# Thin and long MLP tasks in alternation over the border between two batches

## The chip, the cores and the metric

The kernel runs on one core of one Trainium2 chip. Its time is the device time of that core in microseconds (us). The engines are named as the profile names them: PE is TensorE's matrix multiply, PEld its weight load, DVE is VectorE, ACT is ScalarE, POOL is GpSimd, and SP is SyncE, which issues most transfers.

## The reference, cut to what matters

Three models in a row, all in float32:

```python
# attention, 4 batches x 8 heads, 576 rows, head size 64
scores = scale * q @ k.T
scores = where(scores >= max(scores) - tau, scores, -1e9)
x = softmax(scores) @ v                      # joined to x[b, 576, 512]
# mixer MLP, one batch after the other
u  = x + (U, V applied over the 576 rows of x)   # rank 32
z  = u + relu(u @ w_ch1) @ w_ch2             # 512 -> 2048 -> 512
# routed experts
logits = z @ w_gate; local_gate = sigmoid(z @ w_local)
e = argmax(logits), or the row before's expert if local_gate >= 0.5
out = softmax(logits)[e] * (relu(z @ w1[e]) @ w2[e])
```

## The kernel before, in words

**Two streams in one loop.** The attention works on pairs of heads (16 pairs, four to a batch), and each pair takes nine steps. Step n therefore belongs to pair p = n // 9, with j = n % 9. Steps 0 to 35 (batch 0) run alone. From step 36 on the MLP of the batch before is woven in: `FILL[n]` lists the MLP tasks of step n. The attention ends with step 143; the steps after it hold only MLP tasks, three to a step. Then comes the routing of all rows to experts, and the experts.

**The tasks.** `mlp_tasks` writes the order of the 82 tasks of a batch. The 576 rows are cut in two stretches, k = 0 with 256 and k = 1 with 320, and the 2048 hidden values in four quarters r. A task computes one bank of PSUM:

- `token_mix`: one task, the first rank-32 product. `mixed` (k, c): the second product plus x, giving u in four blocks c of 128 channels.
- `hidden` (k, r, q): 12 matmuls over u. `channel` (k, r, c): 12 matmuls over the quarter's hidden values, added to z. These are the long tasks; a batch has 32 of each kind, sixteen per k.
- `gate` (k), `logits` (k): the router's products and their transposes. `rows` (i): the five row blocks of z, transposed for storing.

`gate`, `logits`, `rows` and `mixed` are the thin tasks. In the order before, all of a batch's long tasks are done, then `gate` and `logits` of both k, three `rows`, the next batch's `token_mix`, the last two `rows`, and the eight `mixed`, and then the next `hidden`.

**Two banks.** Task t writes bank t % 2 of `mlp_banks`. TensorE waits before task t until ACT and DVE have emptied bank t % 2 of task t - 2 (L663, L664). `hidden` is emptied by ACT (L839) and then DVE (L976), `channel` by DVE (L984), `mixed` by two ACT copies (L836, L837) and DVE (L973), `gate` by ACT (L844), `logits` by DVE (L989), `rows` by ACT (L851). Further waits: `gate` waits for the last `channel` of its k (L699), the first `hidden` of a k for all `mixed` of that k (L682).

**The order on each engine in step n**, written out by hand (L740 to L765, L887 to L913, L1017 to L1038):

- PE: scores of step n + 1 (after ACT's copy `et_copied` of step n - 1), now and then the value product, `turn_out` or `turn_part`, the first MLP task, `turn(n)`, the other MLP tasks.
- ACT: exponential and limit of n + 1, denominators (j = 3, 8), the first task's copy, `copy_turned(n)`, `copy_out` and `copy_part` at some j, the other tasks' copies.
- DVE: minimum and mask of n + 1, `inverse` and `write_x` at j = 1 and 5, then all tasks of the step.

The weight pieces of the MLP pass through a ring of six, which POOL splits (L468, L473) when the last user of a slot is done; the steps for this (`SPLIT_AT`) and for the first expert's weights (`FIRST_LOAD`, `FIRST_UPPER`) follow from the task order.

Of the kernel before, what the change touches and what calls it, by code (L numbers as in the profile page):

```python
# [4 lines left out]
F32 = mybir.dt.float32  # L5
# [21 lines left out]
SCALE = DH ** -0.5  # L27
ROWS = [P] * (NT - 1) + [REST]
# [21 lines left out]
SPLIT_ROWS = 3  # L50


def mlp_tasks():

    tasks = []
    for b in range(B):
        rows = [(b, "rows", 0 if i < BLOCKS[0][1] else 1, i, 0) for i in range(NT)]
        tasks.append((b, "token_mix", 0, 0, 0))
        if b:
            tasks += waiting  # L60
        tasks += [(b, "mixed", k, 0, c) for k in range(2) for c in range(KC)]
        for r in range(NQ):
            for k in range(2):
                tasks += [(b, "hidden", k, r, q) for q in range(QUARTER)]
                tasks += [(b, "channel", k, r, c) for c in range(KC)]
        tasks += [(b, "gate", k, 0, 0) for k in range(2)]
        tasks += [(b, "logits", k, 0, 0) for k in range(2)]
        tasks += rows[:SPLIT_ROWS]
        waiting = rows[SPLIT_ROWS:]
    return tasks + waiting  # L70


TASKS = mlp_tasks()
# [5 lines left out]
def emptied(by, t):  # L79

    return sum(by[:t + 1])


def tasks_by_step():
# [3 lines left out]
    for n in range(ALONE, NBLK):  # L88
        b, at = divmod(n, ALONE)
        if b == 1:  # L90
            want = 0 if at == 0 else 1 if at == 1 else 3 if at in (6, 15, 17, 26) else 2
        else:
            want = 4 if at == 0 else 3 if at in (3, 5, 6, 8, 15, 17, 24, 26) else 2
        plan.append(list(range(done, done + want)))
        done += want
    assert done == INDEX[B - 2, "channel", 1, NQ - 1, KC - 1] + 1
# [41 lines left out]
SPARE = 80  # L138


def attention_and_mlp(nc, ctx, keep, A, first_weights):
# [18 lines left out]
    o_cols = sb("o_cols", [P, PAD])  # L160
    u4 = sb("u4", [P, NT, 4, RANK])
    v4 = sb("v4", [P, S], F32R)
    stat = sb("stat", [P, 4, 2])
# [13 lines left out]
    w_gate = sb("w_gate", [P, KC, P // KC])  # L177
# [4 lines left out]
    g4 = hid_hi[:, 0:2, :].rearrange("p a b -> p (a b)")[:, 0:D]  # L182
# [98 lines left out]
    CLEARS = 17  # L281
# [142 lines left out]
    def gpsimd(pool):  # L424
        done = 0
        for buf in (raw_q[0:REST, :, NT - 1, 1], raw_q[REST:P, :, NT - 1, 0], raw_k[REST:P, :, NT - 1], ident[:], first_k[DH:P, 0:2].bitcast(F32), first_k[0:DH, 2:4].bitcast(F32),
                    raw_v[REST:P, 0, NT - 1], raw_v[REST:P, 1, NT - 1], ex[:, :, S:PAD], u4[REST:P, NT - 1], x[REST:P, NT - 1], gates[:], w_gate[:], z[:, KC * S:], o_cols[:, S:PAD], least[:], den[:]):
# [121 lines left out]
    def tensor(pe):  # L549
# [101 lines left out]
        def turn_out(p, k):  # L651
            pe.wait_ge(o_copied, 2 * p + k + 1)
            for n, c in enumerate(range(*BLOCKS[k])):
                last = nc.tensor.transpose(aux[:, 512 * k + n * P:512 * k + (n + 1) * P], o_cols[:, c * P:(c + 1) * P], ident[:])
# [1007 lines left out]
```

## Time and profile before

| | |
|---|---|
| median of 3 runs | 1121.52 us (1120.58 to 1122.43) |
| the profiled execution's own time | 1121.17 us |
| its span, first to last instruction | 1119.4 us |
| PE busy | 1052.2 us, 94% of the span |
| DVE, ACT, POOL busy | 512.8, 469.2, 367.9 us |
| mean granted TensorE clock | 0.982 of full speed |
| chain that ended last | 85% PE, 4% ACT, 3% DVE, 3% DMA |

A task's time on PE is best read from start to start: the ends of matmuls are modelled and overlap the next start. Border 1 is the stretch in which batch 0's MLP ends and batch 1's begins, border 2 and border 3 the next two. Borders 1 and 2 lie in the part with attention (steps 72 to 78 and 108 to 114); border 3 (steps 144 to 150) and the end of the MLP (steps 171 to 174) lie after it.

### The profile page before, as it was taken

To read this page: it belongs to the slowest core of one execution; us is meant where nothing else is said; L and a number is where in the kernel's file an instruction comes from. 1 tells how busy PE (TensorE), PEld (TensorE's weight loads), DVE (VectorE), ACT (ScalarE), POOL (GpSimd) and SP (SyncE) were. 2 spreads that over 40 slices of the span, in tenths; PEclk is the share of its full clock that TensorE was granted. 3 is DMA by queue.
4 is the path that set the end of the run, shared out by engine and by line. 5 is a ranking of instruction groups with operands and counts; after the bars stand their busy time and mean duration, and the time that the engine had idled before them with its cause. 6 is when DMAs were issued, how large, how long until landed. Compare 5 with 4: busy or idle time off the path is not lost.

```text
span 1119.4 us, 19936 instructions
## 1 busy us (share of the span) xinstructions
PE 1052.2 (94%) x7054; PEld 917.3 (82%) x7055; DVE 512.8 (46%) x1000; ACT 469.2 (42%) x894; POOL 367.9 (33%) x340
## 2 busy tenths in 40 slices
PE   6999899999889999988999998999869999999995
PEld 5766889999679999967999996999757887887784
DVE  4665544545444454545445452222463543335731
ACT  5776534444554443455444343122213442334620
POOL 4455122643403264340326422378110121111111
PEclk9999999999999999999999999999959999999998
DMA  7887051614434361543325113331254533245510
GB/s 165 194 184 186 20 138 46 169 60 118 145 74 95 93 166 49 128 139 80 80 86 144 49 37 120 122 132 39 71 179 142 187 122 124 72 154 185 183 42 31
DMA packets 110649, 127.26 MB, mean 114 GB/s; under 512 B 67213, under 2 KB 67213, under 8 KB 110544
## 3 DMA queue, kind: packets, MB, share of 16 engines
q1 hardware_dynamic: 104480, 114.54, 36.0%
q0 software_dynamic: 3520, 10.75, 3.0%
q8 instruction: 63, 1.03, 0.4%
q10 hardware_dynamic: 2544, 0.59, 0.2%
q14 instruction: 42, 0.34, 0.1%
HBM read 87.90 MB, written 10.22 MB: 88 GB/s over the span
## 4 chain that ended last, share of the span: by engine, by line
PE 85%; ACT 4%; DVE 3%; DMA 3%; issue 3%; SPq 1%; POOL 1%; POOLq 0%; ACTq 0%; DVEq 0%
PE mlp_banks L696 18%; PE mlp_banks L688 18%; PE p_down L1353 11%; PE p_up L1353 8%; PE aux L646 7%; PE score_banks L622 6%; PE score_banks L629 6%; DMA xg<-mlp_rows,gather_at 2%; PE p_turn L1373 1%; PE aux L589 1%; PE p_x L1346 1%; DMA mlp_rows<-z_rows 1%; ACT et_first L814 1%; DVE stat L928 1%; PE mlp_banks L671 1%
## 5 line engine op out<-in xcount | busy, mean ns | idle before, releaser
L788 ACT ACTIVATE ex<-score_banks,stat 128x576 f32<-128x576 f32 x132 | 97.8, 741 | 178.0 <-DVE stat L928 178.0
L468 POOL CAST w_hi<-stage 128x1024 fp32r<-128x1024 f32 x64 | 66.6, 1041 | 288.2 <-PE mlp_banks L688 240.8
L688 PE MATMUL mlp_banks<-u_hi,w_hi 128*128 128x320 f32 (+1 forms) x512 | 157.0, 307 | 3.7 <-ACT u_hi L837 3.3
L696 PE MATMUL mlp_banks<-hid_hi,w_hi 128*128 128x320 f32 (+1 forms) x512 | 158.5, 310 | 0.9 <-DVE hid_lo L976 0.9
L937 DVE SCALAR_TENSOR_TENSOR ex<-score_banks,stat,ex 128x576 f32<-128x576 f32 x132 | 107.7, 816 | 106.6 <-ACT stat L792 105.7
L473 POOL TENSOR_TENSOR w_lo<-stage,w_hi 128x1024 fp32r<-128x1024 f32 (+1 forms) x70 | 154.0, 2202 | 4.8
L688 PE MATMUL mlp_banks<-u_hi,w_lo 128*128 128x320 f32 (+1 forms) x512 | 151.3, 296 | 0.0
L696 PE MATMUL mlp_banks<-hid_lo,w_hi 128*128 128x320 f32 (+1 forms) x512 | 151.3, 296 | 0.0
L696 PE MATMUL mlp_banks<-hid_hi,w_lo 128*128 128x320 f32 (+1 forms) x512 | 151.3, 296 | 0.0
L688 PE MATMUL mlp_banks<-u_lo,w_hi 128*128 128x320 f32 (+1 forms) x512 | 151.3, 295 | 0.0
L1353 PE MATMUL p_down<-weights,hid_upper 128*128 x336 | 111.9, 404 | 5.7 <-issue 5.7
L1353 PE MATMUL p_up<-weights,x_upper 128*128 x336 | 111.7, 404 | 3.5 <-issue 1.8
L976 DVE SCALAR_TENSOR_TENSOR hid_lo<-mlp_banks,hid_hi 128x256 fp32r<-128x256 f32 (+1 forms) x128 | 58.4, 456 | 113.4 <-ACT hid_hi L839 112.8
L928 DVE TENSOR_REDUCE stat<-score_banks 128x1 f32<-128x576 f32 x132 | 99.4, 753 | 22.9 <-PE score_banks L622 14.2
L839 ACT ACTIVATE hid_hi<-mlp_banks 128x256 fp32r<-128x256 f32 (+1 forms) x128 | 52.3, 409 | 135.4 <-PE mlp_banks L688 134.9
L984 DVE TENSOR_TENSOR z<-mlp_banks,z 128x256 f32<-128x256 f32 (+1 forms) x128 | 58.4, 457 | 110.5 <-PE mlp_banks L696 110.5
L622 PE MATMUL score_banks<-k_tiles,q_tiles 128*128 128x288 f32 x552 | 98.0, 303 | 7.9 <-ACT et_first L814 5.4
L696 PEld LDWEIGHTS mlp_banks<-hid_hi,w_hi 128*128 128x128 f32 x512 | 96.8, 189 | 6.1 <-issue 3.3
L688 PEld LDWEIGHTS mlp_banks<-u_hi,w_hi 128*128 128x128 f32 x512 | 96.8, 189 | 5.2 <-ACT u_hi L837 3.5
L1294 POOL DMA_INDIRECT out<-x,scatter_at x21 | 21.5, 1022 | 234.7 <-DVE x L1575 234.7
L696 PEld LDWEIGHTS mlp_banks<-hid_lo,w_hi 128*128 128x128 f32 x512 | 97.0, 190 | 0.0
L688 PEld LDWEIGHTS mlp_banks<-u_lo,w_hi 128*128 128x128 f32 x512 | 97.0, 190 | 0.0
(231 smaller groups left out, 1950.4 us busy)
## 6 DMA issues: line engine op xcount, KB each, us to landing
stage<-in_moe_w_ch SPq DMA_DIRECT2D x64, 512.0 KB, 3.7
w_raw<-in_moe_w SPq DMA_DIRECT2D x64, 512.0 KB, 5.2
q_tiles<-q_parts SPq DMA_DIRECT2D x30, 320.0 KB, 4.3
q_tiles<-q_parts SPq DMA_DIRECT2D x60, 160.0 KB, 4.2
k_tiles<-k_parts SPq DMA_DIRECT2D x60, 144.0 KB, 3.5
raw_q<-in_q SPq DMA_DIRECT2D x32, 128.0 KB, 3.2
raw_v<-in_v SPq DMA_DIRECT2D x32, 128.0 KB, 2.8
raw_k<-in_k SPq DMA_DIRECT2D x28, 128.0 KB, 2.7
```

Of the source, the lines that this page charges most:

```text
L468: nc.gpsimd.tensor_copy(w_hi[:, n % RING], stage[:, n % 2]).then_inc(w_upper, 1)
L473: last = nc.gpsimd.tensor_tensor(w_lo[:, n % RING, cols], stage[:, n % 2, cols], w_hi[:, n % RING, cols].bitcast(F32), ALU.subtract)
L622: last = nc.tensor.matmul(score_of(n)[:, a], q_tiles[:, s, 2 * m + t, i * P:(i + 1) * P], k_tiles[:, s, m, a * HALF:(a + 1) * HALF], start ...
L629: last = nc.tensor.transpose(turned_of(n)[:, c], ex[:, n % 3, c * P:(c + 1) * P], ident[:])
L646: last = nc.tensor.matmul(aux[h * DH:(h + 1) * DH, 512 * k:512 * k + w], raw_v[:, p % 2, c, h], et[k][:, h, c], start=(c == 0), stop=(c == ...
L688: last = nc.tensor.matmul(bank[:, 0:w], ch1(a, g, d, c), of[:, d, cols], start=(d == 0 and n == 0), stop=(d == KC - 1 and n == 2))
L696: last = nc.tensor.matmul(bank[:, 0:w], ch2(a, g, q, c), of[:, q, 0:w], start=(q == 0 and n == 0), stop=(q == QUARTER - 1 and n == 2))
L788: nc.scalar.activation(ex_of(n), score_of(n), ACT.Exp, bias=stat[:, n % 4, 0:1], scale=-1.0).then_inc(exp_done, 1)
L928: nc.vector.tensor_reduce(stat[:, n % 4, 0:1], score_of(n), AX.XY, ALU.min).then_inc(row_min, 1)
L937: nc.vector.scalar_tensor_tensor(out=ex_of(n), in0=score_of(n), scalar=stat[:, n % 4, 1:2], in1=ex_of(n), op0=ALU.is_le, op1=ALU.mult, acc ...
L976: nc.vector.scalar_tensor_tensor(out=hid_lo[:, c, 0:w], in0=bank[:, 0:w], scalar=0.0, in1=hid_hi[:, c, 0:w].bitcast(F32), op0=ALU.max, op1 ...
L1353: last = nc.tensor.matmul(to, a, weights[:, bass.ds(at_w + b + c * step, 512)], start=(c == 0 and k == 0), stop=(c == len(rows) - 1 and k ...
```

## The change

The second half of a batch's last quarter (k = 1, r = 3) is held back. Its four `hidden` take turns with `gate`, `logits` and two `rows` of k = 0; its four `channel` take turns with the next batch's `mixed` of k = 0; and `gate`, `logits` and three `rows` of k = 1 take turns with the next batch's first four `hidden`. In every batch, the batch alone at the start too, the first four `channel` of k = 0 take turns with the `mixed` of k = 1. `g4`, which `token_mix` writes, gets a buffer of its own instead of lying over `hid_hi`. The list of tasks per step changes with it; the MLP has 177 steps in all instead of 175. In batches 1 and 2 of the loop some steps hold three or four tasks (`FIRST_STEPS`). A few pads are not cleared any more (15 instead of 17 clears), the gate's stationary operand has 16 columns per block instead of 32, and the last row block of some transposes 64 rows instead of 128.

For the last batch there is no next one: after its last `hidden` (k = 1, r = 3) with the thin tasks of k = 0 between them come four `channel`, `gate`, `logits` and three `rows`, one after the other.

```diff
-SPLIT_ROWS = 3
+def taking_turns(*lists):
+    return [task for row in itertools.zip_longest(*lists) for task in row if task is not None]
...
-        if b:
-            tasks += waiting
-        tasks += [(b, "mixed", k, 0, c) for k in range(2) for c in range(KC)]
+        tasks += taking_turns(left[:KC], quarter("mixed", 0, 0))
+        tasks += taking_turns(left[KC:], quarter("hidden", 0, 0))
+        tasks += taking_turns(quarter("channel", 0, 0), quarter("mixed", 1, 0))
         for r in range(NQ):
             for k in range(2):
-                tasks += [(b, "hidden", k, r, q) for q in range(QUARTER)]
-                tasks += [(b, "channel", k, r, c) for c in range(KC)]
-        tasks += [(b, "gate", k, 0, 0) for k in range(2)]
-        tasks += [(b, "logits", k, 0, 0) for k in range(2)]
-        tasks += rows[:SPLIT_ROWS]
-        waiting = rows[SPLIT_ROWS:]
-    return tasks + waiting
+                if (r, k) not in ((0, 0), (NQ - 1, 1)):
+                    tasks += quarter("hidden", k, r) + quarter("channel", k, r)
+        tasks += taking_turns([gate[0], logits[0]] + rows[:BLOCKS[0][1]], quarter("hidden", 1, NQ - 1))
+        ends.append(len(tasks))
+        left = quarter("channel", 1, NQ - 1) + [gate[1], logits[1]] + rows[BLOCKS[0][1]:]
+    return tasks + left, ends
...
+FIRST_STEPS = (2, 2, 3, 4, 2, 3, 2, 3, 3, 2, 2, 2)
...
         if b == 1:
-            want = 0 if at == 0 else 1 if at == 1 else 3 if at in (6, 15, 17, 26) else 2
+            want = min(at, 2)
         else:
-            want = 4 if at == 0 else 3 if at in (3, 5, 6, 8, 15, 17, 24, 26) else 2
+            want = FIRST_STEPS[at] if at < len(FIRST_STEPS) else 3 if at in (15, 20, 25, 30) else 2
...
-    o_cols = sb("o_cols", [P, PAD])
+    o_cols = sb("o_cols", [P, S])
+    g4 = sb("g4", [P, D], F32R)
...
-    w_gate = sb("w_gate", [P, KC, P // KC])
+    w_gate = sb("w_gate", [P, KC, GATES])
...
-    CLEARS = 17
+    CLEARS = 15
...
             elif kind == "logits":
+                pe.wait_ge(act_task, emptied(BY_ACT, INDEX[b, "gate", k, 0, 0]))
...
+                if k == 1 and b < B - 1:
+                    act.wait_ge(rows_stored[0], 16 * (3 * b + 1))
+                    act.wait_ge(rows_stored[1], 16 * (2 * b + 1))
                 nc.scalar.copy(gate_part[:, START[k]:START[k] + w], bank[:, 0:w]).then_inc(act_task, 1)
```

The steps of the changed plan that the prediction speaks of, in the kernel's names (b is the batch whose MLP it is; border 1 shown, border 2 is 36 steps later):

```
70 gate k0, hidden k1 r3 c0          77 gate k1, hidden k0 r0 c0 (b+1), logits k1
71 logits k0, hidden c1              78 hidden c1 (b+1), rows 2
72 rows 0, hidden c2                 79 hidden c2, rows 3, hidden c3
73 rows 1, hidden c3                 80 rows 4, channel k0 r0 c0, mixed k1 c0
74 token_mix, channel c0, mixed c0   81 channel c1, mixed k1 c1
75 channel c1, mixed c1, c2, c2      82 channel c2, mixed k1 c2
76 channel c3, mixed c3              83 channel c3, mixed k1 c3; 84 hidden k1 r0 c0
```

## Rows read from the trace of the kernel before

**Rows 1.** PE's waits over the whole span: waited for, us, times, longest

```profile
PE mlp_banks L676 <- ACT z_rows L851: 3.9, 3, 1.7
```

**Rows 2.** Stretch, us; busy PE, PEld, DVE, ACT, POOL; PE clock, DMA share, GB/s

```profile
288.44:323.31 34.87, 27.86 (x190) 20.99 (x190) 14.70 (x34) 20.21 (x49) 7.34 (x6) 0.95 0.56 145
323.31:485.24 161.93, 161.59 (x1238) 150.83 (x1238) 77.96 (x170) 69.20 (x152) 64.23 (x43) 1.00 0.37 98
485.24:518.52 33.28, 26.26 (x190) 20.23 (x190) 14.70 (x34) 20.22 (x49) 7.34 (x6) 1.00 0.57 152
677.76:698.10 20.34, 16.46 (x104) 11.40 (x103) 5.05 (x14) 9.62 (x25) 4.18 (x3) 1.00 0.34 110
```

**Rows 3.** Timeline of PE in border 2, and one value product of border 1

```profile
490.18 0.60 PE L709 MATMUL mlp_banks<-ident,z 128*128 128x128 f32 x4
490.62 0.71 PE L629 MATMUL score_banks<-ident,ex 128*128 128x128 f32 x5
...
494.37 4.46 PE L671 MATMUL mlp_banks<-x,u 128*128 128x512 f32 x10
498.26 1.09 PE L622 MATMUL score_banks<-k_tiles,q_tiles 128*128 128x288 f32 x4
...
503.99 2.38 PE L646 MATMUL aux<-et_first,raw_v 128*64 128x256 f32 x20
506.29 0.39 PE L676 MATMUL mlp_banks<-v,hid_hi 128*128 128x256 f32 x1
...
506.96 0.71 PE L629 MATMUL score_banks<-ident,ex 128*128 128x128 f32 x5
...
307.52 3.64 PE L646 MATMUL aux<-et_first,raw_v 128*64 128x256 f32 x20
```

**Rows 4.** Timeline of PE in a dense step: turn, long task, scores

```profile
571.84 0.71 PE L629 MATMUL score_banks<-ident,ex 128*128 128x128 f32 x5
572.31 0.36 PE L696 MATMUL mlp_banks<-hid_hi,w_hi 128*128 128x256 f32 x1
...
573.82 0.69 PE L622 MATMUL score_banks<-k_tiles,q_tiles 128*128 128x288 f32 x4
574.34 0.28 PE L696 MATMUL mlp_banks<-hid_hi,w_hi 128*128 128x256 f32 x1
```

**Rows 5.** Timeline of a thin step of border 1, all engines

```profile
295.67 0.79 PE L622 MATMUL score_banks<-k_tiles,q_tiles 128*128 128x288 f32 x4 [0.70 <-ACT et_first L814]
...
296.50 0.76 DVE L928 TENSOR_REDUCE stat<-score_banks 128x1 f32<-128x576 f32 x1 [0.35 <-PE score_banks L622]
...
297.29 0.74 ACT L788 ACTIVATE ex<-score_banks,stat 128x576 f32<-128x576 f32 x1 [0.62 <-DVE stat L928]
...
298.25 0.82 DVE L937 SCALAR_TENSOR_TENSOR ex<-score_banks,stat,ex 128x576 f32<-128x576 f32 x1 [0.99 <-ACT stat L792]
298.58 0.71 ACT L814 ACTIVATE et_first<-score_banks 128x640 f32<-128x640 f32 x1
```

**Rows 6.** Timeline without attention: a k = 1 hidden's emptying

```profile
788.68 0.31 PE L688 MATMUL mlp_banks<-u_hi,w_hi 128*128 128x320 f32 x1
...
788.88 0.44 ACT L839 ACTIVATE hid_hi<-mlp_banks 128x320 fp32r<-128x320 f32 x1 [7.25 <-PE mlp_banks L688]
...
789.35 0.49 DVE L976 SCALAR_TENSOR_TENSOR hid_lo<-mlp_banks,hid_hi 128x320 fp32r<-128x320 f32 x1 [1.81 <-ACT hid_hi L839]
```

**Rows 7.** Timeline of the end of the MLP and of the routing

```profile
801.09 1.49 PE L701 MATMUL mlp_banks<-z,w_gate 128*32 128x256 f32 x16
...
804.06 0.32 DVE L1458 TENSOR_REDUCE c<-gates 128x20 f32<-128x160 f32 x1
...
804.13 3.25 ACT L851 COPY x<-mlp_banks 128x512 f32<-128x512 f32 x5 [1.07 <-PE mlp_banks L709]
...
808.89 1.34 DVE L1477 TENSOR_TENSOR_SCAN won<-kept,p_up 32x576 f32<-32x576 f32 x1
```

**Rows 8.** Busy time from 306 to 312 us, columns as in rows 2

```profile
306.00:312.00 6.00, 6.00 (x37) 4.04 (x38) 1.91 (x4) 2.37 (x7) 0.00 (x0) 0.72 0.82 187
```

## The prediction on record

> **What bounds the kernel now.** I read the share of busy time first: PE works 94% of the span, so only PE's own gaps can be won. The list of waits then says where they are: nearly all that are not at the start or in the routing belong to thin tasks around a border, such as `mixed` waiting 3.9 us in three places for a `rows` copy [rows 1]. Third, the windows [rows 2]: between borders 1 and 2 PE is busy 161.59 of 161.93 us, in the three borders 27.86 of 34.87, 26.26 of 33.28 and 16.46 of 20.34. Busy time is flattering, since modelled ends cover part of each gap, so I count work from start to start. A `rows` task takes 0.44 and `token_mix` 3.9 us; the k = 0 value product takes 2.3 and a k = 0 `mixed` 0.67 [rows 3]; in a dense stretch `turn` takes 0.47, a k = 0 long task 1.51 and the scores 0.52 [rows 4]; a k = 1 long task takes 1.76 and a k = 1 `mixed` about 0.76 (320 columns for 256).
>
> Border 2 by these: 6 scores 3.1, 7 turns 3.3, `token_mix` 3.9, value product 2.3, five `rows` 2.2, eight `mixed` 5.7, `gate` and `logits` about 1.9, `turn_out` and `turn_part` about 1.2 (the last two by their counts of matmuls): 23.6 of 33.28 us, so 9.7 are lost. Border 1 has the same work and loses 11.3; 1.3 of the difference is its value product, 3.64 instead of 2.38 us [rows 3], in a stretch whose granted clock is 0.72 on average, partly the 1.2 GHz level [rows 8], behind a gap of 1.7 us on PE [rows 1]. Border 3 has 14.4 of work in 20.34 us and loses 5.9. That is 27 us in sight. The question is how much of it comes back.
>
> **What ends a wait now.** Two chains set the least length of a step. From the scores' start (295.67) it is 0.83 to the minimum, 0.79 to the exponential, 0.96 to the mask's start, 0.82 to its end: 3.40 us, and only then does DVE turn to the step's tasks [rows 5]. ACT comes to a first task's copy 2.45 us after the scores' start and to `copy_turned` after that, which the scores after next need: 3.62 us from the scores' start to that copy's end in this step, with a `rows` copy in front (295.67 to 299.29). Without attention, a k = 1 `hidden` is out of its bank 1.16 us after the next task starts (788.68 to 789.84) [rows 6]; a `channel`, without the ACT copy, 0.69; k = 0 about 1.05 and 0.62. PE's first matmul after a wait costs another 0.1.
>
> **The change, attention borders (1 and 2).** The same tasks and the same matmuls; what alters is the cover. I walk steps 70 to 84 with these durations, each engine in its own order, and note where PE must wait:
> - Steps 70 to 76. `gate` k0 now directly follows the last `channel` of its k: 0.2 beyond the scores that cover it. Steps 71 and 72 are short (3.2 of PE work), so scores wait 0.4 for `copy_turned`. `token_mix` is well covered, its emptying by `channel` c0. Step 75 holds four tasks: `channel` c2 needs `channel` c1 out of its bank, but DVE reaches it only behind the mask, 4.4 after the scores' start, where PE is at 3.6: 0.9.
> - Steps 77 to 80. Each has one or two long tasks with a thin one between, 3.6 to 4.4 us of PE work a step. Scores wait 0.4, 0.3 and 0.7 for `copy_turned`; `hidden` c1 waits 0.3 and c3 0.8 for the `hidden` two tasks before; in step 80 `mixed` waits 0.9 for the `rows` 4 copy, behind exponential, limit and denominators on ACT.
> - Steps 82 to 84. Scores wait 0.3, 0.4 and 0.2, `turn_part` 0.3 for `copy_part`; `channel` c3 waits 0.7 for c2, behind mask and `write_x` on DVE; and `hidden` k1 c0 waits 1.3, because it needs the `mixed` just before it, where before eight long tasks lay between.
>
> That sums to 8.1, with some seven restarts 8.8 us a border, beside 9.7 and 11.3, to which 0.2 is added in both for a wait two steps behind the old borders. Border 2 gains 1.1 and border 1 2.7, if the half clock stays away: **-3.8**. The bounds of a border's loss: 4.6 if the bank waits vanish (then only ScalarE's loop, the `mixed` wait and a few tenths are left), and 10 or more if the DVE queue slips further.
>
> **Border 3, without attention.** Nothing stands between the tasks any more but the tasks. A `hidden` behind a thin task waits for the `hidden` before it: emptying 1.05 to 1.16 plus restart 0.1, minus the thin task's 0.33 to 0.44, so 0.75 to 0.85 each. There are four of these with the next batch's first `hidden` and the following `channel` (0.85 + 3 x 0.75 = 3.1), two more in steps 143 and 145 that `turn` or `turn_out` covers partly (1.0), `hidden` k0 c0 behind `gate` waits 0.8 for `mixed` c3, `hidden` k1 c0 waits 1.7 for `mixed` k1 c3. `channel` beside `mixed` is nearly free (0.69 against 0.67), 0.2, and the change of operand type costs 0.08 on seven long tasks, 0.6. Sum 7.4 beside 5.9: **+1.5**.
>
> **End of the MLP.** Before, `gate` and `logits` of k = 0 fitted into waits that k = 1 has anyway: from 801.09 to the routing's first instruction at 804.06 [rows 7]. This end stays as long. Ahead of it, though, now stand `gate` 0.57, `logits` 0.33 and two `rows` 0.86, which before lay in that wait or behind `logits` under the routing; plus the wait of `gate` for the `channel` just before it 0.8 and three `hidden` waits 1.0 + 0.9 + 0.9, and 0.1: 5.3. Back comes part: ACT has three `rows` copies instead of five (3.25 us from 804.13) ahead of the exponential and copy that the scan at 808.89 waits for, 0.9 [rows 7]. **+4.4**. Bounds: +1.7 if the `hidden` waits were covered, +5.3 if the scan gained nothing.
>
> **Batch 0.** `mixed` k1 moves from steps 40 and 41 to 42 to 45. The old place loses about 2.5 there; the new one has three short steps (3.3 of PE work) with scores waits of 0.25, 0.25 and 0.7, and a `hidden` k1 wait of 0.85, with restarts 2.7: **+0.2**.
>
> **Free parts.** Fewer clears sit before POOL's idle time; 16 instead of 32 stationary columns and 64 instead of 128 change no column that streams; `g4`'s own buffer removes no wait seen. Transfers keep their place relative to their users: a `rows` 2 store has two steps until `rows` 4 needs the buffer, POOL's splits and SP's loads, the experts' first weights too, move together with the last user of their slot. If POOL were late, the next `channel` would show it first.
>
> **Sum.** -3.8 + 1.5 + 4.4 + 0.2 = +2.3 us on the profiled execution's 1121.17 gives 1123.5. The median of the runs is 0.35 above that execution: 1123.8 us.
>
> **A rule weighed.** The two-bank rotation hides an emptying only as long as the task in between: 1.16 us against 0.44 [rows 3, 6]. The Trainium skill, Perfetto Trace Analysis, section Matmuls, says that independent matmul groups should rotate through banks so that the emptying of one overlaps the next group. If that held in full here, all bank waits would go. By rows: 4.6 instead of 8.8 at two borders, 4.1 less at border 3, 2.7 less at the end, so 1108.6 us; I give it 0.05 within the first rival below.
>
> **Rivals.**
> - Faster (0.25): the bank waits at borders 1 and 2 are covered because delayed scores leave DVE time for the step's tasks. Loss 4.6 each, a gain of 12.2 where I count 3.8: 1115.4 us. For it speaks that borders 1 and 2 lose most in waits behind one `rows` copy [rows 1], which long tasks do cover; against it that DVE takes tasks strictly behind the mask. It is faster by over 0.2% from a loss of about 6.5 a border downwards.
> - Slower by more (0.20): the slips of steps 77 to 84 add up, or PE falls to 1.2 GHz in one of them as it did at 306 [rows 8]. The borders lose what they did, and only the +6.1 of the rest stays: 1127.6.
> - Nothing comes of it (0.15): waits only change places, and the end, too, is covered: 1121.5.
> - My forecast (0.40), its own range 1121.8 to 1125.8, half within 0.2% and half above.
>
> **Chances.** 0.2% (2.2 us) is about what a measurement can tell from no change. Faster 0.25; same 0.15 + 0.18 = 0.33; slower 0.22 + 0.20 = 0.42. The range reaches from the faster rival's number to the slower one's, 1115.5 to 1127.5, and leaves about 0.2 out.
>
> **What would show it.** After the change: waits of L688 for `hid_lo` (L976) of 0.7 to 1.0 us around border 3 and at the end; one of over 1 us for `mixed` (L973) before `hidden` k1 in every batch; no wait of `mixed` for a `rows` copy over 1 us, except 0.9 at step 80; border windows from step 70 to 84 with 8 to 9 us more than their work; a clock of 1.00 there; the routing's first instruction at 804.06 + 5.3 + 1.5 + 0.2 - 3.8 = 807.3 us. It is wrong if the borders lose under 6.5 each, or if the end moves the routing by less than 3.

## The result, and the profile after

The changed kernel takes 1127.07 us (median of 20 runs, 1124.96 to 1128.95) beside 1121.84 us for the kernel before (20 runs, 1119.89 to 1127.75): ratio 1.0042, 95% interval 1.0033 to 1.0051. It is slower, by some 4.7 us by the ratio and 5.2 between the medians. The forecast was 1123.8, slower by 2.3, with a range from 1115.5 to 1127.5: the measured time lies at the upper end of it.

The profiled execution has a span of 1124.4 us beside 1119.4, with the same clock over the whole, 0.983 and 0.982. Line numbers have moved: `hidden` is L702 now, `channel` L710, `mixed` L690 and L692, `gate` L715, `logits` L720; the copies are L854 (`hid_hi`), L994 (`hid_lo`), L862 (`gate`) and L869 (`rows`).

PE's waits over the whole span, which answer to [rows 1] (waited for, us, times, longest):

```profile
PE mlp_banks L702 <- DVE hid_lo L994: 3.9, 8, 0.7
PE mlp_banks L702 <- DVE u_lo L991: 3.6, 4, 1.5
...
PE mlp_banks L710 <- ACT u_hi L852: 1.6, 2, 0.8
PE mlp_banks L702 <- ACT x L869: 1.4, 2, 0.7
PE mlp_banks L690 <- ACT z_rows L869: 1.4, 2, 0.7
...
PE mlp_banks L715 <- DVE z L1002: 1.3, 2, 0.7
```

The wait of `mixed` for a `rows` copy has gone from 3.9 to 1.4 us, as the change means it to. The first two rows are what took its place: a `hidden` that wants its bank while DVE still empties the `hidden` two tasks before, and a k = 1 `hidden` that wants the last `mixed`. Where these waits stand is shown by PE's timeline, rows with an idle time only. Border 2 (border 1 is the same 194.2 us earlier):

```profile
493.15 0.39 PE L710 MATMUL mlp_banks<-hid_hi,w_hi 128*128 128x320 f32 x1 [0.79 <-ACT u_hi L852]
...
514.10 0.36 PE L702 MATMUL mlp_banks<-u_hi,w_hi 128*128 128x256 f32 x1 [0.67 <-DVE hid_lo L994]
519.42 0.41 PE L690 MATMUL mlp_banks<-v,g 128*128 128x320 f32 x1 [0.70 <-ACT z_rows L869]
...
537.54 0.38 PE L702 MATMUL mlp_banks<-u_hi,w_hi 128*128 128x320 f32 x1 [0.84 <-DVE u_lo L991]
```

Border 3, without attention (the last row is `hidden` k1 c0 behind `mixed` k1 c3):

```profile
689.83 0.35 PE L702 MATMUL mlp_banks<-u_hi,w_hi 128*128 128x256 f32 x1 [0.69 <-DVE hid_lo L994]
692.52 0.36 PE L702 MATMUL mlp_banks<-u_hi,w_hi 128*128 128x256 f32 x1 [0.58 <-DVE hid_lo L994]
695.21 0.35 PE L702 MATMUL mlp_banks<-u_hi,w_hi 128*128 128x256 f32 x1 [0.59 <-DVE hid_lo L994]
...
709.17 0.38 PE L702 MATMUL mlp_banks<-u_hi,w_hi 128*128 128x320 f32 x1 [1.47 <-DVE u_lo L991]
```

The end of the MLP, PE's timeline, and DVE's for one `hidden`, the routing's first instruction and the scan, which answer to [rows 7]:

```profile
787.16 0.62 PE L715 MATMUL mlp_banks<-z,w_gate 128*16 128x256 f32 x8 [0.61 <-DVE z L1002]
790.88 0.38 PE L702 MATMUL mlp_banks<-u_hi,w_hi 128*128 128x320 f32 x1 [0.92 <-DVE gates L1007]
794.03 0.38 PE L702 MATMUL mlp_banks<-u_hi,w_hi 128*128 128x320 f32 x1 [0.71 <-ACT x L869]
796.53 0.49 DVE L994 SCALAR_TENSOR_TENSOR hid_lo<-mlp_banks,hid_hi 128x320 fp32r<-128x320 f32 x1 [2.65 <-ACT hid_hi L854]
797.17 0.39 PE L702 MATMUL mlp_banks<-u_hi,w_hi 128*128 128x320 f32 x1 [0.70 <-ACT x L869]
806.88 0.73 PE L715 MATMUL mlp_banks<-z,w_gate 128*16 128x320 f32 x8 [0.67 <-DVE z L1002]
808.24 0.52 PE L720 MATMUL mlp_banks<-ident,z_rows 128*128 128x128 f32 x3 [0.63 <-ACT z_rows L862]
...
809.16 0.32 DVE L1476 TENSOR_REDUCE c<-gates 128x20 f32<-128x160 f32 x1
813.10 1.34 DVE L1495 TENSOR_TENSOR_SCAN won<-kept,p_up 32x576 f32<-32x576 f32 x1 [0.48 <-ACT kept L1422]
```

The brackets of the three `hidden` name the event that came last before them, the emptying of the thin task just before. By the program each waits for the `hidden` two tasks before: DVE ends that one's emptying at 797.02 (796.53 + 0.49), and PE starts at 797.17.

The routing begins at 809.16 instead of 804.06 and its scan at 813.10 instead of 808.89. Nearly the whole loss is in place by then.

### The profile page after: what moved, and what is told of

The parts are those of the page before. It is cut to its first block, busy times and chain, and to the rows that moved or that the text cites. A ratio compares the mean times of both kernels' runs of the same rounds, so it can differ in the third digit from the quotient of the medians.

```text
span 1124.4 us, 19937 instructions
## 1 busy us (share of the span) xinstructions
PE 1054.0 (94%) x7054; PEld 917.0 (82%) x7055; DVE 510.7 (45%) x1000; ACT 471.2 (42%) x894; POOL 367.2 (33%) x338
## 4 chain that ended last, share of the span: by engine, by line
PE 78%; SPq 6%; DVE 5%; issue 4%; ACT 4%; DMA 3%; POOL 1%; POOLq 0%; DVEq 0%; ACTq 0%
PE mlp_banks L710 18%; PE mlp_banks L702 17%; PE p_down L1371 11%; PE p_up L1371 8%; PE aux L660 6%; PE score_banks L636 5%; PE score_banks L643 5%; DMA xg<-mlp_rows,gather_at 2%; PE mlp_banks L685 2%; PE p_x L1364 1%; PE p_turn L1391 1%; PE aux L603 1%; DVE stat L946 1%; PE mlp_banks L692 1%; DVE hid_lo L994 1%
## 5 line engine op out<-in xcount | busy, mean ns | idle before, releaser
L702 PE MATMUL mlp_banks<-u_hi,w_hi 128*128 128x320 f32 (+1 forms) x512 | 158.6, 310 | 10.9 <-DVE hid_lo L994 3.9
L710 PE MATMUL mlp_banks<-hid_hi,w_hi 128*128 128x320 f32 (+1 forms) x512 | 158.4, 309 | 3.8 <-ACT u_hi L852 1.6
L702 PE MATMUL mlp_banks<-u_hi,w_lo 128*128 128x320 f32 (+1 forms) x512 | 151.4, 296 | 0.0
L710 PE MATMUL mlp_banks<-hid_hi,w_lo 128*128 128x320 f32 (+1 forms) x512 | 151.3, 296 | 0.0
L702 PE MATMUL mlp_banks<-u_lo,w_hi 128*128 128x320 f32 (+1 forms) x512 | 151.3, 295 | 0.0
L710 PE MATMUL mlp_banks<-hid_lo,w_hi 128*128 128x320 f32 (+1 forms) x512 | 151.2, 295 | 0.0
L994 DVE SCALAR_TENSOR_TENSOR hid_lo<-mlp_banks,hid_hi 128x256 fp32r<-128x256 f32 (+1 forms) x128 | 58.4, 456 | 153.3 <-ACT hid_hi L854 153.0
L854 ACT ACTIVATE hid_hi<-mlp_banks 128x256 fp32r<-128x256 f32 (+1 forms) x128 | 52.4, 409 | 143.3 <-PE mlp_banks L702 143.1
L702 PEld LDWEIGHTS mlp_banks<-u_hi,w_hi 128*128 128x128 f32 x512 | 96.8, 189 | 18.4 <-issue 6.1
L710 PEld LDWEIGHTS mlp_banks<-hid_hi,w_hi 128*128 128x128 f32 x512 | 96.8, 189 | 8.8 <-issue 3.5
L710 PEld LDWEIGHTS mlp_banks<-hid_lo,w_hi 128*128 128x128 f32 x512 | 97.0, 189 | 0.2 <-issue 0.2
L702 PEld LDWEIGHTS mlp_banks<-u_lo,w_hi 128*128 128x128 f32 x512 | 97.0, 189 | 0.0
```

Of the source, the lines that this page charges most:

```text
L702: last = nc.tensor.matmul(bank[:, 0:w], ch1(a, g, d, c), of[:, d, cols], start=(d == 0 and n == 0), stop=(d == KC - 1 and n == 2))
L710: last = nc.tensor.matmul(bank[:, 0:w], ch2(a, g, q, c), of[:, q, 0:w], start=(q == 0 and n == 0), stop=(q == QUARTER - 1 and n == 2))
L994: nc.vector.scalar_tensor_tensor(out=hid_lo[:, c, 0:w], in0=bank[:, 0:w], scalar=0.0, in1=hid_hi[:, c, 0:w].bitcast(F32), op0=ALU.max, op1 ...
```

## How the runs are compared

A row of the timeline says when a piece of work begins, so the stretch between two such rows holds a known set of tasks. I cut each profiled execution at seven rows: the scores that PE computes in step 37 (those of step 38; below and in the expectations "the scores of step 37"); `hidden` k1 r0 c0 of batches 0, 1, 2 and 3 (written h0 to h3); the routing's first instruction; and PE's first gather of rows (`p_x`), behind the routing. Up to h3 the MLP tasks in each stretch are the same for all orders; at the end the new order puts two `rows` ahead of the routing which otherwise lie behind it. The attention's steps in it are the same for all kernels with the changed plan of steps; with the plan of before, one or two steps fall into the stretch beside it. The kernels are described in the two sections on experiments. Stretches in us:

```
                     37-h0   h0-h1   h1-h2   h2-h3  h3-rout.  -p_x   -end
before               43.63  197.78  195.21  170.74   94.27   25.77  289.6
rest_only            43.64  196.24  195.27  170.53   94.28   25.83  289.8
plan_only            44.31  196.60  194.97  169.62   94.34   25.73  289.5
after                44.75  195.74  194.20  171.63   99.99   24.96  290.3
only_end             43.65  196.23  196.80  170.61   99.86   24.97  294.3
end_undone           44.78  195.77  194.24  171.63   94.38   25.83  291.4
border3_end_undone   44.80  195.76  194.22  170.40   94.31   25.83  291.3
mixed_first          44.87  194.31  192.70  170.18   99.96   24.97  292.6
hybrid               44.32  194.30  192.67  171.33   94.30   25.82  292.1
before_banks4        43.67  196.24  195.27  166.94   94.30   25.42  289.7
banks4               44.80  195.75  194.22  167.22   96.92   24.97  289.4
hybrid_banks4        44.31  194.30  192.69  166.01   94.29   25.49  293.2
held3_banks4         44.33  194.31  192.69  165.74   94.42   25.48  289.7
first_banks4         44.89  194.31  192.68  165.70   96.89   24.97  290.9
```

Where two kernels have the same instructions in a stretch, it repeats to a few hundredths (h3 to the routing: 94.27 to 94.42 in the nine kernels with the old end), except for the last column, for two stretches over an old border, 197.78 and 196.80, and for h2 to h3 with the old border 3 (169.6 to 171.3), of which more below.

## Experiments: which part costs what

**The old order with all other edits (`rest_only`).** The order of tasks and the plan of steps are those of before; `g4`'s own buffer, the narrower gate weights and transposes, the fewer clears and the extra wait of `logits` stay (the extra wait of `gate`'s copy for earlier stores goes with the new order). In this and all further kernels `HELD[b]` says whether batch b's last quarter is held back, and `MIX[b]` where batch b's `mixed` of k = 1 go: all ahead (`early`), in turns behind a `channel` (`turns`), or in turns ahead of it (`first`). Against the changed kernel:

```diff
+HELD = (False, False, False, False)
+MIX = ('early', 'early', 'early', 'early')
...
+        else:
+            tasks += waiting + quarter("mixed", 0, 0)
+            if MIX[b] == "early":
+                tasks += quarter("mixed", 1, 0)
+            tasks += quarter("hidden", 0, 0)
+        if MIX[b] == "early":
+            tasks += quarter("channel", 0, 0)
...
+        else:
+            tasks += gate + logits + rows[:3]
+            left, waiting = [], rows[3:]
...
-            want = FIRST_STEPS[at] if at < len(FIRST_STEPS) else 3 if at in (15, 20, 25, 30) else 2
+            want = 4 if at == 0 else 3 if at in (3, 5, 6, 8, 15, 17, 24, 26) else 2
```

> The old order of tasks and the old list of steps, with all other edits of the change (own buffer for g4, 16 stationary columns in the gate, 64 rows in the last transposes, 15 clears). Theory (only the order costs): within 1 us of the kernel before, ratio 0.999 to 1.001, and the routing's first instruction (the reduction over gates) at 804 us as before. Rival (the small edits cost part of it): 2 us or more slower.

Measured: 1122.08 us (12 runs) beside 1122.11, ratio 1.0000 (0.9987 to 1.0013). The free parts are free as far as this interval of 1.5 us each way can tell, and the loss is in the order of tasks or its plan of steps.

**The new end alone (`only_end`).** `rest_only`, but the last batch's `gate`, `logits` and two `rows` of k = 0 take turns with its last quarter of `hidden`.

```diff
-HELD = (False, False, False, False)
+HELD = (False, False, False, True)
```

> As rest_only, but the last batch alone is in the new order at its end: thin tasks of k = 0 between the four hidden of k = 1, then four channel, gate, logits and three rows. Theory (the end is what costs): gate, logits and two rows are put ahead of the routing (1.8 us), one wait of gate and three of hidden for a bank are new (3.6 us), 0.9 us come back in front of the scan: 4.5 to 5 us slower than before, ratio 1.004; the routing's first instruction 5.3 us later than in rest_only. Rival (the end is hidden, the loss sits at the three borders): under 2 us slower.

Measured: 1129.30 us (6 runs), ratio 1.0060 (1.0040 to 1.0081). From h3 to the routing it takes 99.86 us instead of 94.28, and 24.97 instead of 25.83 from there to `p_x`: +5.6 and -0.9. PE's timeline has the waits of the changed kernel, one after the other:

```profile
788.29 0.63 PE L729 MATMUL mlp_banks<-z,w_gate 128*16 128x256 f32 x8 [0.61 <-DVE z L1016]
792.02 0.38 PE L716 MATMUL mlp_banks<-u_hi,w_hi 128*128 128x320 f32 x1 [0.93 <-DVE gates L1021]
795.15 0.38 PE L716 MATMUL mlp_banks<-u_hi,w_hi 128*128 128x320 f32 x1 [0.71 <-ACT x L883]
798.29 0.38 PE L716 MATMUL mlp_banks<-u_hi,w_hi 128*128 128x320 f32 x1 [0.71 <-ACT x L883]
```

The sum, 4.7, is most of the 7.2 us in its median. In its profiled execution 1.5 us more lie in border 2 and 4.5 behind the routing, both in the clock (last sections).

**The end undone (`end_undone`).** The changed kernel with the old end for the last batch.

```diff
+HELD = (True, True, True, False)
+MIX = ('turns', 'turns', 'turns', 'turns')
```

> The changed kernel with the old order at the end of the last batch alone. Theory: 4.5 to 5 us faster than the changed kernel, so level with the kernel before (ratio 0.999 to 1.001). Rival (the loss sits at the borders): still 3 us or more slower than before.

Measured: 1123.12 us (12 runs), ratio 1.0003 (0.9987 to 1.0019). The stretch to the routing is back at 94.38, the next at 25.83. So from both sides the end costs 4.7 us in the stretches; in the times of the runs it is 4.4 by the ratios (1.0042 to 1.0003) and 3.9 between the medians. Without it the change is no longer slower by anything that can be measured. Nor is it faster.

**Border 3 and the end undone (`border3_end_undone`).** Only borders 1 and 2 keep the new order, and the last batch has `mixed` k1 in its old place.

```diff
+HELD = (True, True, False, False)
+MIX = ('turns', 'turns', 'turns', 'early')
```

> The changed kernel with the old order at the end and at border 3, the two stretches without attention; borders 1 and 2 and batch 0 stay new. Theory (alternation pays where attention steps stand between the tasks, and costs where none do): 1.5 to 3 us faster than end_undone, ratio to before 0.997 to 0.9985. Rival (border 3 is even): as end_undone.

Measured: 1121.72 us (12 runs), ratio 0.9993 (0.9980 to 1.0006); h2 to h3 170.40 us instead of 171.63. Border 3 in the new order costs 1.2 us beside this kernel. That is less than the 1.5 to 3 us that I expected, and the ratio is above the expected 0.997 to 0.9985: with `mixed` in turns behind `channel`, the new order at borders 1 and 2 is no gain that the runs can tell.

**The plan of steps alone (`plan_only`).** The old order, put on the steps of the changed plan: each border stands two steps later, and more tasks stand behind the attention's end. By difference, 1.3 us were missing in the account. Against `rest_only`:

```diff
-            want = 0 if at == 0 else 1 if at == 1 else 3 if at in (6, 15, 17, 26) else 2
+            want = min(at, 2)
...
-            want = 4 if at == 0 else 3 if at in (3, 5, 6, 8, 15, 17, 24, 26) else 2
+            want = FIRST_STEPS[at] if at < len(FIRST_STEPS) else 3 if at in (15, 20, 25, 30) else 2
```

> The order of tasks of before with the steps of the changed plan (and all the other edits): every border stands two steps later, and two steps' more tasks stand behind the end of the attention. What the forecast left out costs, by difference, about 1.3 us between batch 2's hidden k1 and batch 3's, beside the attention of two steps that lies in front of that stretch instead of in it. Theory that the plan's shift at the attention's end is this cost: from batch 2's hidden k1 to batch 3's within 0.3 us of border3_end_undone's 170.4 us, which has the same steps and the same order there; and the whole to batch 3's hidden k1, from the scores of step 37, 1 to 2 us longer than the 605.7 us of rest_only, ratio 1.000 to 1.003. Rival that the shift costs nothing and the held quarter is what costs: 605.7 us again, and 169 us or less from batch 2's hidden k1 to batch 3's.

Measured: 1122.87 us (12 runs), ratio 1.0002 (0.9987 to 1.0016). My theory fell, and the rival holds in the main, though its stretch is 169.62 and not the 169 or less that it asked for. From the scores of step 37 to h3 it takes 605.50 us, as `rest_only` does (605.68), and h2 to h3 is not the 170.4 that I expected. The shift costs nothing. The 0.8 us between this and `border3_end_undone`, which has the same tasks and steps there, is mostly one transfer. In `border3_end_undone`, ACT's timeline:

```profile
687.91 0.58 ACT L886 COPY z_rows<-mlp_banks 64x512 f32<-64x512 f32 x1 [2.30 <-DMA mlp_rows<-z_rows]
```

and in `plan_only`:

```profile
688.50 0.58 ACT L886 COPY z_rows<-mlp_banks 64x512 f32<-64x512 f32 x1 [1.58 <-PE mlp_banks L709]
```

The `rows` 4 copy waits for an earlier store to leave its buffer in the one and not in the other; PE's next `mixed` then waits 1.37 instead of 0.65 us. Why that store lands later was not tried. `hybrid` (below) has the same tasks there once more and takes 171.33: its copy waits 2.54 us and its `mixed` 1.61, and behind that wait the clock falls, which takes another 0.75 us (from that `mixed` to h3 20.56 us, beside 19.81 in `plan_only`). PE's row, and the window of the fall (the clock is the third number from the end):

```profile
686.29 0.38 PE L707 MATMUL mlp_banks<-v,g 128*128 128x256 f32 x1 [1.61 <-ACT z_rows L886]
688.00:692.00 4.00, 3.77 (x18) 3.52 (x17) 1.12 (x3) 2.01 (x6) 0.00 (x0) 0.57 0.00 1
```

With `plan_only` the parts can be compared at equal steps, for the order alone: batch 0 +0.44, border 1 -0.86, border 2 -0.77, h2 to h3 +2.01, the end +5.65 and -0.77.

## Experiments: what the waits are made of, and a better version

**`mixed` first (`mixed_first`).** The changed kernel, but in taking turns `mixed` k1 goes ahead of `channel` k0, so that a long task lies between the last `mixed` and `hidden` k1 c0.

```diff
+HELD = (True, True, True, True)
+MIX = ('first', 'first', 'first', 'first')
...
+        elif MIX[b] == "turns":
+            tasks += taking_turns(quarter("channel", 0, 0), quarter("mixed", 1, 0))
+        else:
+            tasks += taking_turns(quarter("mixed", 1, 0), quarter("channel", 0, 0))
```

> The changed kernel with one edit: where the first four channel of k = 0 and the mixed of k = 1 take turns, mixed goes first, so that a channel stands between the last mixed and the hidden of k = 1 that needs it. Theory: the wait of that hidden (0.5, 0.8, 0.8 and 1.5 us in the four batches, with restarts 4.0) goes, and at borders 1 and 2 the wait for the rows copy in step 80 (0.7 each) too: 4 to 5.5 us faster than the changed kernel, ratio to before 0.999 to 1.0005. Rival (the wait only changes place): less than 1.5 us faster.

Measured: 1123.94 us (12 runs), ratio 1.0003 (0.9987 to 1.0020), 3 us less than the changed kernel and not the 4 to 5.5 expected. Its rows of `hidden` k1 c0 at h1 and at h3 show no idle time any more, but the wait for the `rows` 4 copy, which was to go too, has grown from 0.70 to 1.38 us (here border 2):

```profile
342.04 0.31 PE L719 MATMUL mlp_banks<-u_hi,w_hi 128*128 128x320 f32 x1
...
518.08 0.39 PE L727 MATMUL mlp_banks<-hid_hi,w_hi 128*128 128x256 f32 x1 [1.38 <-ACT z_rows L886]
...
704.92 0.38 PE L719 MATMUL mlp_banks<-u_hi,w_hi 128*128 128x320 f32 x1
```

There the bank of `rows` 4 goes to `channel` c0 with only a `mixed` in between, where before it was a `channel`. Borders 1, 2 and 3 are still 1.43, 1.50 and 1.45 us shorter. At border 2 that is 2.15 us less from the scores behind this place to h2 (520.25 to 537.54, and 519.60 to 534.74) and 0.65 more before them. Of the 2.15, 1.08 is idle time that has gone (0.84 of `hidden` and 0.24 of `channel` c3); the rest shows only from start to start, and which row it belongs to was not tried. Batch 0 gains nothing (44.87 beside 44.75), and the last column of the table is 2.3 us longer, by the clock (last section).

**Four banks behind the attention (`banks4`, `before_banks4`).** The scores' banks are free once the attention has ended. From the first multiple of four at or behind step 146's first task on, the tasks rotate over four banks, and a task waits for the one four before it; the last four use two again, because the routing takes banks. `banks4` is the changed order, `before_banks4` the old one.

```diff
+    def task_bank(t):
+        n = t % 4 if WIDE <= t < len(TASKS) - 4 else t % 2
+        return mlp_banks[:, 512 * n:512 * n + 512] if n < 2 else score_banks[:, 0, 512 * (n - 2):512 * (n - 1)]
...
-                pe.wait_ge(act_task, emptied(BY_ACT, t - 2))
-                pe.wait_ge(dve_task, emptied(BY_DVE, t - 2))
+                back = 4 if WIDE + 4 <= t < len(TASKS) - 2 else 2
+                pe.wait_ge(act_task, emptied(BY_ACT, t - back))
+                pe.wait_ge(dve_task, emptied(BY_DVE, t - back))
+            if t == WIDE + 2:
+                pe.wait_ge(et_copied, NBLK)
```

> The changed kernel, its order untouched, but from the step after the attention's last value product on (border 3 and the end) the tasks rotate over four banks instead of two: two of the attention's, free by then, join. Theory (border 3 and the end lose in bank waits): the hidden waits of 0.5 to 0.9 us with 0.1 each go, five at border 3 and three at the end, 4 to 5 us faster than the changed kernel; the wait of hidden k1 for mixed (1.5) and those of gate for channel (0.6) stay. Rival (the waits are for data, not banks): under 1.5 us faster.

> The old order with the same four banks after the attention. Theory: its border 3 loses 5.9 us in a row of thin tasks on two banks, of which 3 to 5 come back; at the end gate and logits wait for data, so nothing there: 3 to 5 us faster than before, ratio 0.9955 to 0.9975. Rival (ACT's copies bound the thin tasks whatever the banks): under 1.5 us faster.

Measured: 1120.41 us (12 runs), ratio 0.9982 (0.9964 to 1.0001), and 1120.00 us (12 runs), ratio 0.9972 (0.9955 to 0.9989). In the changed order h2 to h3 falls from 171.63 to 167.22 and h3 to the routing from 99.99 to 96.92, 7.5 us together where 4 to 5 were expected. In `banks4` the three waits of `hidden` for a bank at 790 to 797 are gone; what is left ahead of the routing are waits for data:

```profile
782.84 0.62 PE L740 MATMUL score_banks<-z,w_gate 128*16 128x256 f32 x8 [0.61 <-DVE z L1027]
...
799.53 0.73 PE L740 MATMUL score_banks<-z,w_gate 128*16 128x320 f32 x8 [0.68 <-DVE z L1027]
800.89 0.52 PE L745 MATMUL mlp_banks<-ident,z_rows 128*128 128x128 f32 x3 [0.63 <-ACT z_rows L887]
```

The 2.6 us by which this end still exceeds the old one's 94.3 go, by my sum and not by a run of its own, to the thin tasks themselves (1.8) and `gate`'s wait for `channel` (0.6 of idle time): they stand in front of the routing, whatever the banks. The old border 3 gains 3.6 us from four banks (170.53 to 166.94), the new one 4.4.

**The new order only where attention covers it (`hybrid`).** Borders 1 and 2 new, with `mixed` first; border 3, batch 0's beginning, the last batch and the end old; two banks.

```diff
+HELD = (True, True, False, False)
+MIX = ('early', 'first', 'first', 'early')
```

> New order at borders 1 and 2 alone, with mixed before channel; batch 0, border 3 and the end in the old order, two banks. Theory: against border3_end_undone (1121.7 us) 3 to 4 us less, so about 1118, ratio to before 0.9960 to 0.9975. Rival (the alternation gains nothing under the attention either): 0.998 or more.

Measured: 1119.18 us (12 runs), ratio 0.9968 (0.9954 to 0.9982). Borders 1 and 2 take 2.3 us less each than in `plan_only`; that is what the idea is worth, with the two tasks in the better turn. It is not all that is there: the wait of 1.38 us for the `rows` 4 copy stands in both (1.37 in this trace).

**The best of both (`hybrid_banks4`, `held3_banks4`, `first_banks4`).** `hybrid` with four banks; the same with border 3 new as well, and `mixed` first for the last batch; the whole new order, end included, with `mixed` first and four banks.

```diff
 hybrid_banks4
+HELD = (True, True, False, False)
+MIX = ('early', 'first', 'first', 'early')
 held3_banks4
+HELD = (True, True, True, False)
+MIX = ('early', 'first', 'first', 'first')
 first_banks4
+HELD = (True, True, True, True)
+MIX = ('first', 'first', 'first', 'first')
```

> The order of hybrid (borders 1 and 2 in the new order, mixed k1 ahead of channel k0 there, border 3 and the end as before) with the MLP's banks rotating over four from the end of the attention on, as in before_banks4. Theory that the two gains lie in different places (hybrid's 2.2 us in borders 1 and 2, the four banks' 3.9 us in border 3 and the first tasks behind the attention): batch 3's hidden k1 starts near 703 us instead of 709.1, the routing's first instruction near 797.5 instead of 803.4, ratio 0.994 to 0.996. Rival that both win the same waits around border 3: routing near 799.5, ratio 0.997.

> As hybrid_banks4, but border 3 too in the new order (mixed k1 first), the end of the MLP as before. Theory that the new order is no loss once four banks cover a long task's emptying behind a thin one: batch 3's hidden k1 within 1 us of hybrid_banks4's, on either side, and from there 94.3 us to the routing in both. Rival that border 3 in the new order costs its 1.2 us (end_undone against border3_end_undone) with four banks too: 1.2 us later, ratio 0.001 higher.

> The changed kernel with both repairs: mixed k1 ahead of channel k0 in every batch, and four banks behind the attention; border 3 and the end stay in the new order. mixed_first brought batch 3's hidden k1 to 704.9 us and banks4 to 704.9, from 709.2 both; together I expect 701 to 703. From there to the routing 96.9 us as in banks4, 2.6 more than the old end's 94.3. Ratio 0.996 to 0.998, and about 0.002 above held3_banks4, if the end's thin tasks ahead of the routing are what is left of its price; equal to it if four banks had covered that too.

Measured, 6 runs each beside 1122.89 us: 1112.73 us, ratio 0.9904 (0.9880 to 0.9928); 1112.41 us, 0.9904 (0.9882 to 0.9926); 1115.93 us, 0.9932 (0.9909 to 0.9954). The first two beat both kernels by some 10 and 15 us, more than I expected (ratio 0.994 to 0.996); the third was expected at 0.996 to 0.998. In the stretches the gains add: `held3_banks4` beside `rest_only` has -1.9, -2.6 and -4.8 from h0 to h3, 0.7 more in batch 0, and -0.2 around the routing, 8.8 in all. Border 3's order makes no difference with four banks (166.01 and 165.74). The end does: 96.89 us instead of 94.42, and 3.5 us in the medians of the last two.

## Why the prediction was off

The sign and the places were right; the sizes all leaned to the good side. The measured 1127.1 us is closer to the rival "slower by more" (1127.6) than to my 1123.8, but not by that rival's mechanism: it has the borders lose what they did, or the clock fall in them, and they came out 1.6 us shorter at a full clock.

Two sums of the prediction do not come out of their own terms. The terms ahead of the routing, 0.57 + 0.33 + 0.86 + 0.8 + 1.0 + 0.9 + 0.9 + 0.1, make 5.5 and not 5.3. Batch 0's waits, 0.25 + 0.25 + 0.7 + 0.85 with four restarts of 0.1, make 2.45 and not 2.7. The two slips nearly cancel in the total.

Next, what a wait costs. The idle time in brackets understates it. At the end of the MLP, PE's rows of `after` from the last matmul of a `hidden` to the next `hidden`:

```profile
795.72 0.31 PE L702 MATMUL mlp_banks<-u_hi,w_lo 128*128 128x320 f32 x1
795.87 0.60 PE L724 MATMUL mlp_banks<-ident,z 128*128 128x128 f32 x4
797.17 0.39 PE L702 MATMUL mlp_banks<-u_hi,w_hi 128*128 128x320 f32 x1 [0.70 <-ACT x L869]
```

The `rows` task begins at 795.87 and takes 0.44 us where something follows it at once; the `hidden` comes 1.30 behind it. That is 0.86, and the first of its matmuls then takes 0.08 more than the others. From `hidden` to `hidden` it is 3.14 us (794.03 to 797.17), of which 1.76 and 0.44 are work: 0.94 lost, beside 0.70 of idle time and 0.9 in the forecast. Read so, the waits are close to the walk: 1.7 for `hidden` k1 c0 in border 3 (1.7 forecast), 0.7 to 0.9 for its `hidden` waits (0.75 to 0.85), 1.1 for 1.3 + 0.1 before `hidden` k1 in borders 1 and 2.

The terms, beside the order's own cost at equal steps (`after` less `plan_only`):

- **Borders 1 and 2, forecast -3.8, of which 1.3 was the half clock: measured -1.6 without it.** Of the remaining 2.5 (1.4 and 1.1) came 0.86 and 0.77. The windows from h1 to h2, first of `after`, then of `plan_only`, show how little one sees in idle time:

```profile
343.34:537.54 194.20, 189.01 (x1427) 171.27 (x1428) 91.96 (x205) 89.92 (x200) 71.56 (x49) 1.00 0.41 106
```

```profile
344.35:539.32 194.97, 187.92 (x1429) 170.98 (x1428) 92.55 (x205) 89.46 (x200) 71.53 (x49) 1.00 0.42 106
```

  PE's idle time falls by 1.86 us (7.05 to 5.19), and its busy time rises by 1.09 with as many matmuls. A few long waits have become more short ones, each with the two small costs that idle time leaves out. How much a new border still loses against its work, which I put at 8 to 9 us, was not counted over again; only its difference from `plan_only` was.
- **The half clock.** It is a matter of the execution. `rest_only`, with the old order, has the granted clock at 1.00 in both borders (h0 to h1 196.24 where before has 197.78). `only_end` has it fall in its border 2 instead (196.80 for 195.27), again behind a gap of 1.7 us on PE (before the matmul at 501.87). There it costs 1.5 us. But the clock falls in its border 1 too, at 318.0, and there it costs nothing, since slower work fills the next wait. Windows of `only_end` in border 2 and border 1 (the clock is the third number from the end), and the `hidden` behind the second, in `only_end` and in `rest_only`:

```profile
502.00:508.00 6.00, 6.00 (x37) 4.28 (x38) 1.93 (x6) 2.54 (x7) 0.00 (x0) 0.72 0.82 189
317.00:323.00 6.00, 5.78 (x34) 5.70 (x35) 2.89 (x7) 3.59 (x10) 0.00 (x0) 0.72 0.15 34
...
322.48 0.36 PE L716 MATMUL mlp_banks<-u_hi,w_hi 128*128 128x256 f32 x1
...
322.76 0.36 PE L716 MATMUL mlp_banks<-u_hi,w_hi 128*128 128x256 f32 x1 [1.64 <-ACT u_hi L866]
```

  Four of the ten old attention borders in the profiles have such a fall (`before`'s border 1, both of `only_end`, `before_banks4`'s border 2), none of the eighteen new ones, whose longest gap on PE is 1.38 us. Two of the four cost 1.5 us, two are hidden in the next wait. Taken at 1.5 us for each of the two, the old order pays 0.3 us a border for it on average, not 1.3 in one. This is the largest single error: I put what one execution happened to show into the sum as something that the change removes in full.
- **Border 3, forecast +1.5: measured +2.0, or +1.2** beside `border3_end_undone`, whose `rows` 4 copy waits for a store. The waits stand where the walk had them.
- **End of the MLP, forecast +4.4 (5.3 less 0.9): measured +4.9 (5.65 less 0.77).** That "this end stays as long" holds: from the last `channel` matmul to the routing it is 3.26 us (805.90 to 809.16) in `after`, and 3.21 before. Ahead of it the four thin tasks and their four waits come to some 5.6, 0.3 more than the 5.3 that I put into the sum and 0.1 more than its terms make.
- **Batch 0, forecast +0.2: measured +0.4.**
- **Behind the routing, forecast nothing: +0.8** in the profiled execution, from the clock (last section).

The measured terms sum to +6.5 (0.4 - 1.6 + 2.0 + 4.9 + 0.8), the forecast's to +2.3: short by 0.2, 0.9, 0.5, 0.5 and 0.8, and by the 1.3 of the half clock. Against the profiled execution of before it is +5.0 of span: `plan_only`'s span is 0.9 shorter than that one's, and in `after` the attention's start is 0.6 quicker than in `plan_only`.

Of the signs that I named, the `hidden` waits for `hid_lo` and for `mixed` are there, and no `mixed` waits over 1 us for a `rows` copy. The wait for `mixed` before `hidden` k1 is over 1 us only at border 3 (1.47); at borders 1 and 2 it is 0.84 of idle time, in batch 0 0.48. The routing begins at 809.16 and not at 807.3. **The rival of a gain** (borders losing 4.6 each) did not come: at border 2 the waits of `channel` c2 (0.79), of `hidden` c3 (0.67) and for the `rows` copy (0.70) are still there. **The rule on banks** that I weighed, of the Trainium skill, Perfetto Trace Analysis, section Matmuls, was worth what the rows gave for it where it could be put in force: 4.1 us forecast at border 3 and 2.7 at the end, 4.4 and 3.1 measured in `banks4`. In the attention's own borders it was not tried, since the scores hold those banks there.

## What to carry to other kernels

On two banks, a long task behind a thin one waits for the long task before: the thin one covers 0.4 us of an emptying of over 1 us. Thin tasks spread between long ones pay only where other work fills that wait, and the last task of a stage should not be followed at once by its first user. Ask, for each thin task moved forward, whether it lay in a wait that remains: at the end of the MLP it did, and moving it cost its whole length. Count gains in time from start to start, not in idle time, and look at a second execution before a dip of the clock goes into a sum.

## What the hardware showed that I had not expected

**The clock after the routing.** The last column of the table differs by up to 4.8 us between kernels whose instructions there are the same. The granted clock tells why. Windows of before, `after` and `only_end` (stretch; busy PE, PEld, DVE, ACT, POOL; clock):

```profile
836.00:840.00 4.00, 4.00 (x20) 3.25 (x19) 3.35 (x3) 1.27 (x3) 0.00 (x0) 1.00 0.74 221
```

```profile
836.00:840.00 4.00, 3.15 (x8) 2.51 (x9) 1.64 (x2) 2.43 (x3) 1.00 (x1) 0.50 0.21 66
840.00:844.00 4.00, 4.00 (x17) 3.24 (x16) 3.65 (x4) 1.47 (x2) 0.00 (x0) 0.87 0.53 183
```

```profile
840.00:844.00 4.00, 4.00 (x12) 3.09 (x11) 3.89 (x4) 2.56 (x3) 0.00 (x0) 0.54 0.38 119
844.00:848.00 4.00, 3.32 (x19) 2.59 (x18) 0.76 (x2) 1.51 (x2) 0.00 (x0) 1.00 0.94 289
848.00:852.00 4.00, 2.16 (x10) 1.64 (x9) 2.85 (x3) 3.36 (x4) 0.00 (x0) 0.81 0.29 119
852.00:856.00 4.00, 4.00 (x15) 3.20 (x14) 3.68 (x4) 1.45 (x2) 0.00 (x0) 0.76 0.59 197
```

PE drops to the 1.2 GHz level in the routing, where it is busy for 0.8 of the 5 us from 811 in `after`, and rises again when the experts begin. In `only_end` it falls a second time, at 850.5, behind a pause of 1.84 us before PE's matmul at 850.45. The trace of before has the same pause (1.85 us, at 843.92) and no second fall. `hybrid_banks4` shows the same beside `held3_banks4`, with no difference in their instructions there; first the one, then the other:

```profile
836.00:840.00 4.00, 3.74 (x9) 2.97 (x10) 3.88 (x4) 3.25 (x4) 0.00 (x0) 0.50 0.13 40
```

```profile
836.00:840.00 4.00, 4.00 (x19) 3.23 (x18) 3.81 (x4) 1.59 (x2) 0.00 (x0) 1.00 0.53 161
```

It shows in the times: of `hybrid_banks4`'s six runs, two with a mean clock of 0.980 take 1116.6 us and four with 0.983 to 0.985 take 1111.1 to 1112.9; of `hybrid`'s twelve, nine at 0.980 take 1118.7 to 1120.9 and three at 0.982 or 0.983 1116.0 to 1117.4. The fourteen profiles split evenly, and the split goes with the length of the first low stretch: in seven it ends 5.9 to 6.9 us after PE's first gather (`p_x`), there is no second fall, and the last column is 289.4 to 290.3; in the other seven it ends 7.2 to 8.8 us after, there is a second fall, and the column is 290.9 to 294.3. What decides between the two stays open. A difference of up to some 4 us in this kernel can be that alone, which is why the stretches of the table were compared and not the ends.
